# Turning attention outputs into token columns: whole tiles every second stage, or half a tile in every stage

## The reference

```python
batch, n_heads, seq, head_dim = (2, 8, 768, 64)      # n_global 8, n_local 96
scores = scale * np.matmul(q, k.transpose(0, 1, 3, 2)) + bias
scores = np.where(keep, scores, -1000000000.0)
a = np.exp(scores - np.max(scores, axis=-1, keepdims=True))
a = a / (np.sum(a, axis=-1, keepdims=True) + 1e-09)
attn = np.matmul(a, v)                                # then (B, S, H * D) = x

h = x.transpose(0, 2, 1) @ U @ V                      # U (768, 32), V (32, 768)
u = x + h.transpose(0, 2, 1)
x = u + np.maximum(u @ w_ch1, 0.0) @ w_ch2            # 512 -> 2048 -> 512

h = np.maximum(x @ w_in, 0.0); u, v = h[..., :512], h[..., 512:]
v_n = (v - mean(v)) / np.sqrt(var(v) + 1e-06)
out = (u * (w_spatial @ v_n + b_spatial)) @ w_out
```

## Time and profile before

| | us |
|---|---|
| median of 3 runs (507.07 to 509.49) | 507.07 |
| the profiled execution, its own time | 506.97 |
| its span, first to last instruction | 505.0 |
| PE busy in the span | 496.5 (98%) |
| DVE, ACT, POOL busy | 285.8, 213.8, 208.8 |
| attention, from the start to the first product of `hidden` | 97.95 |

### The profile page before, as it was taken

One profiled execution on the slowest core, in us unless ns is written; L12 is line 12 of the kernel. 1 busy time (PEld: TensorE's weight loads), 2 busy tenths in 40 slices (PEclk: granted clock), 3 DMA queues, 4 the chain that ended last, 5 costly groups with the idle time before them and its releaser, 6 DMA issues.

```text
span 505.0 us, 7871 instructions
## 1 busy us (share of the span) xinstructions
PE 496.5 (98%) x2822; PEld 413.9 (82%) x2822; DVE 285.8 (57%) x666; ACT 213.8 (42%) x490; POOL 208.8 (41%) x178
## 2 busy tenths in 40 slices
PE   8999999999999999999999999999999999999997
PEld 7787577787888888888888888888888998889995
DVE  5887688521259376564655565648687356531530
ACT  7978678542235443342342322414654113331121
POOL 6896656354335676744565636423430000000000
PEclk9999999999999999999999999999999999999999
DMA  8810800122222421022222021031500000110002
GB/s 241 282 62 18 298 23 1 45 84 84 83 84 86 165 83 55 30 83 84 83 85 83 1 83 47 27 104 32 177 1 1 1 0 22 43 62 1 1 22 104
DMA packets 14552, 36.28 MB, mean 72 GB/s; under 512 B 2480, under 2 KB 2480, under 8 KB 14512
## 3 DMA queue, kind: packets, MB, share of 16 engines
q1 hardware_dynamic: 12640, 32.35, 18.9%
q10 hardware_dynamic: 1872, 3.41, 1.8%
HBM read 32.61 MB, written 3.15 MB: 71 GB/s over the span
## 4 chain that ended last, share of the span: by engine, by line
PE 93%; ACT 2%; DVE 2%; issue 1%; DMA 1%; SPq 0%; ACTq 0%; DVEq 0%
PE bank L1212 23%; PE bank L1487 15%; PE bank L1419 9%; PE bank L1341 9%; PE bank L1516 9%; PE bank L1509 9%; PE bank L1549 6%; PE bank L1265 4%; PE bank L1247 3%; PE bank L1232 3%; PE bank L1283 1%; ACT prob L944 1%; PE bank L1288 1%; DMA qk_raw<-in_qk 1%; DVE prob L597 1%
## 5 line engine op out<-in xcount | busy, mean ns | idle before, releaser
L462 POOL TENSOR_TENSOR w_slot<-stage,w_slot 128x1024 fp32r<-128x1024 f32 x30 | 73.0, 2444 | 65.6 <-ACT w_slot L1010 65.6
L776 DVE TENSOR_TENSOR uT<-bank,uT 128x512 f32<-128x512 f32 x68 | 45.8, 689 | 25.3 <-PE bank L1516 23.3
L944 ACT ACTIVATE prob<-prob,row_min 128x256 f32<-128x256 f32 (+1 forms) x96 | 46.0, 480 | 13.6 <-DVE row_min L597 13.5
L1212 PE MATMUL bank<-sp_slot,vn 128*128 128x384 f32 x288 | 50.3, 334 | 0.0
L1212 PEld LDWEIGHTS bank<-sp_slot,vn 128*128 128x128 f32 x288 | 50.0, 188 | 0.2
L1487 PE MATMUL bank<-u_op,s_slot 128*128 128x512 f32 x192 | 47.6, 389 | 0.0
L1419 PE MATMUL bank<-hid,w_slot 128*128 128x512 f32 x192 | 47.0, 393 | 0.0
L1341 PE MATMUL bank<-u_split,w_slot 128*128 128x512 f32 x192 | 46.4, 391 | 0.0
L1516 PE MATMUL bank<-hid,w_slot 128*128 128x512 f32 x192 | 46.1, 389 | 0.0
L1509 PE MATMUL bank<-hid,w_slot 128*128 128x512 f32 x192 | 46.1, 389 | 0.0
L1419 PEld LDWEIGHTS bank<-hid,w_slot 128*128 128x128 f32 x192 | 35.7, 188 | 8.2 <-issue 0.9
(11 more groups left out here) (121 smaller groups left out, 832.5 us busy)
## 6 DMA issues: line engine op xcount, KB each, us to landing
stage<-in_w_ch SPq DMA_DIRECT2D x32, 512.0 KB, 3.3
qk_raw<-in_qk SPq DMA_DIRECT2D x23, 256.0 KB, 4.6
v_all<-in_v SPq DMA_DIRECT2D x12, 256.0 KB, 4.9
out_dram<-o_stage ACTq DMA_DIRECT2D x12, 256.0 KB, 2.0
stage<-in_w_spT SPq DMA_DIRECT2D x6, 384.0 KB, 2.9
stage<-in_w_in SPq DMA_DIRECT2D x4, 512.0 KB, 3.9
stage<-in_w_out SPq DMA_DIRECT2D x2, 512.0 KB, 3.5
V_raw<-in_V SPq DMA_DIRECT2D x4, 96.0 KB, 4.4
```

What stands on the lines that cost most here:

```text
L462: nc.gpsimd.tensor_tensor(dst[:, LO, :], stage[n % 2][:, 0:w], dst[:, HI, :].bitcast(F32), ALU.subtract).then_inc(w_lo, 1)
L776: vec.tensor_tensor(y, y_bank(e)[:], y, ALU.add).then_inc(y_sum, 1)
L944: last = sc.activation(prob[r][:, e, 0:w], prob[r][:, e, 0:w], ACT.Exp, bias=row_min[:, k:k + 1], scale=-1.0, accum_out=row_sum[:, q:q + 1])
L1212: last = mm(out_ap, lhs(a), rhs(c), start=(n == 0), stop=(n == 3 * len(terms) - 1))
```

## The change

The tokens are turned by halves of a tile. `turn_x(g)` now does group g's two transposes, into the right half of `aux`, in each stage s from 2 on, for group s-2, right behind `turn_o(s-1)`. `take_xT(g)` copies two columns of blocks in place of four, in each stage, ahead of the exponentials; it also waits for `take_x` of the group turned back in that stage, and `take_x` waits for the `turn_x` behind which it stands. `turn_o(g)` waits for `take_xT(g-2)`. The first four mixes go to `s_bank[0]`; `scores` of groups 18, 20 and 22 wait for their sums, and `turn_o` no longer does. In stages 12 and 13, as in 0 and 1 before, DVE does `take_oT(s)` between the two halves of `score_bias(s+2)` in the same stage, in place of ahead of stage s+1. `round_z(0)` stands at the head of ACT's stage 14. POOL's `split_early(0, 1)` moves from stage 13 to 16, and the fourth `sum_u` from stage 21 to 22. Tile 11's first half is turned behind `turn_o(23)`, its second half in block f = 1. The count of transposes is the same, 48; the copies of ACT are 24 of 256 columns in place of 12 of 512. The code for wide windows, which doesn't run with these inputs, follows.

```diff
@@ -214,7 +214,14 @@
         def mix_bank(j):
+            if j < FIRST:
+                return s_bank[0]
             return o_bank if j >= 2 * KD and j % 2 else aux
+        OT_AMID = (0, 1, 12, 13)
         def globs_before(g):
@@ -524,8 +531,8 @@
                         round_V()
                     if g in (5, 6):
                         split_V(g - 5, g + 3)
-                    if g in (10, 13):
-                        split_early(0, g // 13)
+                    if g in (10, 16):
+                        split_early(0, g // 16)
                     if g in (20, 22):
                         split_early(1, g // 22)
                     if g >= 17 and g % 2:
@@ -629,6 +636,8 @@
                 inv = row_inv[:, g % 2 * 4:g % 2 * 4 + 4]
                 dve.wait_ge(inv_ok, g + 1)
                 dve.wait_ge(o_ps, g + 1)
+                if g:
+                    dve.wait_ge(xT_ps, g)
                 if t == XS:
                     dve.wait_ge(z_acc, 1)
                 cols = slice(hq * 256, hq * 256 + 256)
@@ -706,7 +715,7 @@
             near = windowed(dve)
             with dve.If(near):
                 for s in range(-2, QUADS + 1):
-                    if s >= 3:
+                    if s >= 1 and s - 1 not in OT_AMID:
                         take_oT(s - 1)
                     if 0 <= s < QUADS:
                         take_probT(s)
@@ -716,15 +725,16 @@
                         invert(s)
                     if s == 14:
                         split_z(0)
-                    if s in (0, 1):
+                    if s in OT_AMID:
                         score_bias(s + 2, 0)
                         take_oT(s)
                         score_bias(s + 2, 1)
                     elif 0 <= s + 2 < QUADS:
                         score_bias(s + 2)
-                    if s in (15, 17, 19, 21):
+                    if s in (15, 17, 19):
                         sum_u((s - 15) // 2)
+                    if s == 22:
+                        sum_u(FIRST - 1)
             with dve.Else():
                 dve.sem_inc(w_o, 1)
                 dve.wait_ge(w_tables, 2)
@@ -957,10 +967,14 @@
                     act.wait_ge(pv_done, g - 1)
                 sc.activation(probT[(2 * g + 1) % 4][:, 0:w], pt_bank[1][:, 0:w], ACT.Copy).then_inc(probT_a, 1)
-            def take_xT(t):
-                act.wait_ge(xT_ps, t + 1)
-                sc.activation(uT[:, :, t * P:(t + 1) * P], aux[:].rearrange("p (k t) -> p k t", k=KD),
-                              ACT.Copy).then_inc(xT_sb, 1)
+            def take_xT(g, after=0):
+                t, hq = divmod(g, 2)
+                act.wait_ge(xT_ps, g + 1)
+                if after:
+                    act.wait_ge(x_half, after)
+                sc.activation(uT[:, 2 * hq:2 * hq + 2, t * P:(t + 1) * P],
+                              aux[:, 2 * P:4 * P].rearrange("p (k t) -> p k t", k=2), ACT.Copy).then_inc(xT_sb, 1)
             def copy_z(b):
                 act.wait_ge(z_some, b + 1)
@@ -1017,22 +1031,21 @@
             near = windowed(act)
             with act.If(near):
                 for s in range(-2, QUADS):
+                    if s == 14:
+                        round_z(0)
                     if s >= 2:
                         take_probT(s)
                     if s == 13:
                         copy_z(0)
-                    if s == 14:
-                        round_z(0)
                     if 0 <= s + 1 < QUADS:
                         add_eps(s + 1)
                     if s in (-2, 0, 1):
                         set_bias((0, None, 4, 6)[s + 2])
+                    if s >= 2:
+                        take_xT(s - 2, s)
                     if 0 <= s + 2 < QUADS:
-                        exps(s + 2, 0)
-                    if s >= 2 and s % 2 == 0:
-                        take_xT((s - 2) // 2)
-                    if 0 <= s + 2 < QUADS:
-                        exps(s + 2, 1)
+                        exps(s + 2)
                     if s == -1:
                         set_bias(2)
                     if s in (9, 19):
@@ -1069,8 +1082,10 @@
                     split_stage(2 * f - 7)
                 elif f < 14:
                     split_stage(f + 4)
+                if f == 0:
+                    take_xT(QUADS - 2, QUADS)
                 if f == 1:
-                    take_xT(TILES - 1)
+                    take_xT(QUADS - 1)
                 if f == 4:
                     copy_z(1)
                 if f == 5:
@@ -1223,6 +1238,9 @@
                     pe.wait_ge(biased, 2 * (g - 1))
                 if i >= 2:
                     pe.wait_ge(k_glob, globs_before(g) + 1)
+                if g in (18, 20, 22):
+                    pe.wait_ge(u_sum, (g - 16) // 2)
                 own, keys = slice(i * P, i * P + P), slice(i * P + P - w, i * P + P)
                 for m in range(2):
                     c = heads(g, m)[0]
@@ -1270,22 +1288,21 @@
             def turn_o(g):
-                s = g + 1
                 pe.wait_ge(oT_sb, g + 1)
-                if s % 2:
-                    if s >= 3:
-                        pe.wait_ge(xT_sb, (s - 1) // 2)
-                elif s >= 16:
-                    pe.wait_ge(u_sum, min(s - 14, 8) // 2)
                 if g:
                     pe.wait_ge(x_half, g)
+                if g >= 2:
+                    pe.wait_ge(xT_sb, g - 1)
                 for c in range(2):
                     last = nc.tensor.transpose(aux[:, c * P:(c + 1) * P], oT[g % 2][:, c, :], ident[:])
                 last.then_inc(o_ps, 1)
-            def turn_x(t):
-                for k in range(KD):
-                    last = nc.tensor.transpose(aux[:, k * P:(k + 1) * P], x_all[:, t % XS, k * P:(k + 1) * P],
+            def turn_x(g):
+                t, hq = divmod(g, 2)
+                for c in range(2):
+                    k = 2 * hq + c
+                    last = nc.tensor.transpose(aux[:, (2 + c) * P:(3 + c) * P], x_all[:, t % XS, k * P:(k + 1) * P],
                                                ident[:])
                 last.then_inc(xT_ps, 1)
@@ -1351,8 +1368,10 @@
                         turn(s)
                     if s >= 1:
                         turn_o(s - 1)
+                    if s >= 2:
+                        pe.wait_ge(x_half, s - 1)
+                        turn_x(s - 2)
                     if s == 13:
-                        pe.wait_ge(x_half, 2 * NT)
                         pe.wait_ge(U_in, 16)
                         gather_z(0)
                     if s == 14:
@@ -1360,14 +1379,9 @@
                         fold_z(0)
                     if s + 2 < QUADS:
                         scores(s + 2)
-                    if s >= 2 and s % 2 == 0:
-                        t = (s - 2) // 2
-                        pe.wait_ge(x_half, 2 * t + 2)
-                        turn_x(t)
                     if s in (15, 17, 19, 21):
                         pe.wait_ge(V_split, 2)
                         pe.wait_ge(z_split, 1)
-                        pe.wait_ge(x_half, s)
                         mix((s - 15) // 2)
                     if s == 13:
                         pe.wait_ge(z_copy, 1)
@@ -1375,21 +1389,21 @@
                         pe.wait_ge(z_split, 1)
                     if s >= 0:
                         weigh(s)
-                pe.wait_ge(x_half, QUADS - 1)
                 hidden(0)
                 turn_o(QUADS - 1)
+                pe.wait_ge(x_half, QUADS - 1)
+                turn_x(QUADS - 2)
...
@@ -1431,11 +1442,11 @@
                     hidden(f)
                 if f == 1:
                     pe.wait_ge(x_half, QUADS)
-                    pe.wait_ge(xT_sb, TILES - 1)
+                    pe.wait_ge(xT_sb, QUADS - 1)
                     pe.wait_ge(u_sum, FIRST)
-                    turn_x(TILES - 1)
+                    turn_x(QUADS - 1)
                 if f == 2:
-                    pe.wait_ge(xT_sb, TILES)
+                    pe.wait_ge(xT_sb, QUADS)
                     mix(4)
                 if f == 3:
                     mix_after(6)
```

30 lines of the change are left out of this document (13 added, 17 removed).

## The result

The changed kernel takes 502.78 us, median of 6 runs (502.76 to 502.92); the kernel before took 507.07 beside it. The ratio is 0.9909, with a 95% interval of 0.9893 to 0.9925: 0.8 to 1.1% faster. It goes by the means of the executions, and one of the six of the kernel before took 509.49; the medians alone give 0.9915. The forecast was 503.1, the range 501.9 to 505.0.

A forecast was written before the change was run, and what follows sets the result against it. PE, busy 98% of the span, was taken as the bound. Gains of 0.73+1.56+0.6+1.06 = 3.95, called 4.0, bring the profiled 506.97 to 503.0 and the median to 503.1; range 501.9 to 505.0.

The forecast's parts named there:

- S: S(s) is the start of `scores` in stage s, from which the prediction measures everything.
- 3-9: The span from S(3) to S(9): three pairs of stages, 0.63 won in all.
- 15-21: The span from S(15) to S(21): three pairs of stages, each 7.55 in place of 7.76, 0.6 won.
- The stage: One `scores` to the next, stages 3 to 9: 3.47, DVE's copy to oT latest; lower end 3.38, upper 3.58.
- PE never waits: Rival: a stage takes 3.38, PE's own work; 0.9 more won over about ten stages, 502.2; chance 0.15.
- b: PE's price for entering a kind of work, 0.06, charged also to a group that was waited for.
- The handovers: Rival: two more transposes with their own wait cost 0.1 a stage; only 2.8 won, 504.3; chance 0.13.
- The passage: Stages 11 to 15: 1.56 won since stage 10, bounds 1.0 to 1.9; rival, it stays, 505.1, chance 0.07.
- Moved at no price: POOL's `split_early(0, 1)` in its later place and tile 11's halves were to cost nothing.
- The mixes in another bank cost the same: Stages 15 to 21: moving the mixes' bank adds nothing, and the wait of `scores` for a sum is met.
- The ring through ACT: Rival: PE, DVE and ACT steps in series bind each stage, 0.3 over 20 stages, 509; chance 0.04.
- the step on the end: Stage 22: second half of `weigh` needs ACT, 90.9; `hidden` at 94.0, not 97.95; 1.0 to 1.1 more won.

The follow-up runs named there:

- e8: Changed kernel with DVE's copy to oT ahead of the last of its four passes in all stages where it stood behind it; 502.95 us.
- e1: Changed kernel with DVE's copy to oT in stages 12 and 13 behind all four passes again; 504.04 us.
- e2: Changed kernel with ACT's rounding of z back behind its copy for `weigh` in stage 14; 503.37 us.
- e7: Changed kernel with only the halves, all other parts of the change as before; 506.92 us.
- e6: Kernel before, turning whole tiles, with all other parts of the change; 506.39 us.
- e3: Changed kernel with POOL's `split_early(0, 1)` back in stage 13; 503.43 us.
- e4: Changed kernel with the fourth `sum_u` back in DVE's stage 21; 503.52 us.
- e5: Changed kernel with the first four mixes in `aux` again, with the waits this needs, and the fourth sum back in stage 21; 505.77 us.
- e9: Changed kernel with a second half copy by ACT, into a buffer nobody reads, in stages 4 to 10; 502.86 us.
- e10: Changed kernel with ACT's rounding of the second block of weights moved from stage 19 to ahead of stage 14's exponentials; 502.89 us.
- e11: e8 with ACT's rounding of the second block of weights moved from stage 19 to stage 14; 502.34 us.

## Why the prediction was right, point by point

By its own steps, with S in the profile after:

| step | forecast | measured |
|---|---|---|
| a stage, 3 to 9 | 3.47 | 3.46 |
| 3-9 | 20.82 | 20.76 |
| S(12) | 51.84 | 51.77 |
| `turn_o(12)` | 54.02 | 53.96 |
| S(13), S(14) | 56.01, 59.82 | 55.97, 59.79 |
| S(15) | 63.76 | 63.77 |
| 15-21 | 22.65 | 22.59 |
| `weigh(22)` second half, `turn(23)` | 90.9, 91.5 | 90.86, 91.45 |
| `hidden` | 94.0 | 94.01 |
| in all | 4.0 won | 3.94 by `hidden`, 3.9 by the span |

Of the 3.94, 3.83 is won behind S(3) and 0.11 ahead of it, where the prediction took 0.1; S(3) varies by 0.26 between profiles of the same code, so that 0.11 is not shown. The time came out 0.3 below the forecast because the medians fell by 4.29. The prediction has no term for the 0.2 outside the span; the rest is the spread of the executions.

*The stage.* Right in size and in cause: `turn_o` starts 0.05 behind the end of DVE's copy, and e8, which takes that wait away, brings the 3.38 of PE's own work (3.39 measured). So the rival "PE never waits" named the right bound, 3.38, and was wrong for this kernel only; its price was 0.09 a stage, measured 0.07. The prices of a transpose and of leaving held: the four take 0.53 in e8 (30.09 to 30.62), which is 4 x 0.11 and 0.09, and 0.59 with the lateness. One reading was too strong: not every waited-for group in the rows paid the whole 0.06. The one behind ACT's tile paid 0.03 (27.41 to 27.75 is 0.34), and the prediction itself uses 0.34 for stage 15. And b stands for two things, entering from another kind of work and being late, which cost 0.06 each here; no run shows that they have one cause. The Trainium skill, TensorEngine Tiling (Array Packing), section "Key Properties", says that a change of tiling mode drains TensorE. The rows fit it: `scores` has 64-row tiles, `weigh` 128 x 64, the transposes 128 x 128. No run here measures the drain by itself.

*The handovers.* Two groups back to back, each with its wait, cost no bubble. The rival is refuted by 0.59.

*The passage.* Right to 0.08. e1 shows the early copy to oT in stages 12 and 13 at 1.2, and e2 `round_z` at 0.40, the price named. Of the 1.92 won in 12-15 (2.00 forecast) the halves alone give 0.75 (e7) and the other two parts together 1.17. These two do not add up (e7), and with whole tiles the whole passage wins only 0.47 (e6), since ACT's tile holds `turn_o` there.

*Moved at no price.* Right for `split_early` (e3), and nearly for the fourth sum (e4: 0.09).

*"The mixes in another bank cost the same."* True, and it hides most of the change. Against whole tiles they do cost the same (e6, 15-21: 23.23 to before's 23.24). But the sentence compared with the wrong kernel: halves with the mixes left in `aux` lose 2.7 (e5 less e4). From S(15) to `hidden` they take 33.07 against 31.90 before and 30.24 after. Had I priced the bank as the difference that its absence makes, it would have been the largest single part of these stages.

*The ring through ACT.* Not closed in stages 3 to 9, as forecast, with 0.53 idle (forecast 0.46), and e9 spends half of that for nothing. The prediction charged the half copy its length, 0.35; the next instruction starts 0.27 behind it (e9), and with that the same sum gives 0.54. But in stage 22 ACT is the bound already, as the step on the end had it, and e8 shows how near it is in stage 20.

## What to carry to other kernels

Price a part by the program without it, not by the program before: here the halves alone give -0.17, the rest alone 0.70, and both 3.83, mostly because the halves put a user into a bank that another part had to leave. Of the 3.3 that the two parts win only together, 2.6 lie behind S(15), where the bank is, and 0.7 in 12-15, where an early copy pays only once ACT's tile no longer holds PE. An engine's idle time ahead of a wait is where a movable instruction belongs, and moving it pays only if what it stood before was late by it (e10 nothing, e11 0.5). When a stage shrinks and the time doesn't, follow the lead from stage to stage and read the wait at which it is given back.

## What the runs showed of the hardware

- A group of transposes that comes just after what it waited for takes 0.06 to 0.07 more (0.44 instead of 0.38), with no idle time shown ahead of it. In the six stages from S(3) to S(9) that is 0.4 us (e8) of an engine that looks busy.
- A 128 x 256 copy from an accumulator bank by ACT takes 0.36 to 0.39, and the next instruction may start 0.27 after it (e9); the 512-wide one takes 0.57 to 0.60, and the next may start 0.48 after it (59.92 and 60.40 in e2).
- Some executions are 2.7 us late at the start. The first `scores` took 1.58 in the changed kernel's profile; in e10's, which is such a one, the same 24 matmuls took 2.82. The changed kernel first, then e10:

```profile
6.37 1.58 PE L1250 MATMUL bank<-qk_split 64*128 64x128 f32 x24 [0.18 <-DVE qk_split L587]
```

```profile
6.27 2.82 PE L1252 MATMUL bank<-qk_split 64*128 64x128 f32 x24
9.03 2.50 PE L1221 MATMUL bank<-ident 128*128 128x128 f32 x10
```

The ten fill matmuls behind them took 2.50 instead of 1.38. The first twenty fills, from 1.54 on, took 4.63 in e10 and 4.64 in the changed kernel, 0.23 each in both, so both executions begin at about half pace; the one leaves it by 6.4, the other between 13.2 and 14.6, and from S(3) on the two are equal, though the granted clock reads 1.00 throughout in both. The Trainium skill, TensorE: Matmul & The Clock Gate, section "Part 1: The HAM clock gate (the "warmup" mystery)", says that TensorE starts at 1.2 GHz and goes to 2.4 when it has been busy. The halved pace fits it. But the row of the granted clock does not show it, and PE was just as busy from 1.54 to 6.3 in both, so why one stays slow for some 7 us longer is not shown, and the cause stays open.
